# Attention projections on TensorE: tiles of 64 rows and 128 stationary tokens become tiles of 64 rows and 64 stationary tokens, with a semaphore increment ahead of each unit

## The reference

```python
def phi(x):                                   # x: (4, 8, 576, 64), w_phi: (64, 128)
    proj = np.einsum('bhsd,df->bhsf', x, w_phi)
    proj = proj - np.max(np.abs(proj), axis=-1, keepdims=True)
    return np.concatenate([np.exp(proj), np.exp(-proj)], axis=-1)
q_p, k_p = phi(q), phi(k)
kv = np.einsum('bhsf,bhsd->bhfd', k_p, v); z = np.sum(k_p, axis=2)
out = einsum(q_p, kv) / (einsum(q_p, z) + 1e-6)
```

## Time and profile before

| | |
|---|---|
| median of 3 runs | 886.59 us |
| the 3 runs | 884.9, 886.59, 886.87 us |
| span of the profiled execution | 885.2 us |
| PE busy in it | 98% |
| VectorE, ScalarE, GpSimd busy | 63%, 49%, 34% |
| attention, groups in steady state | one every 10.90 us, until about 174 us |

### The profile page before, as it was taken

How to read it: one execution, slowest core, us unless ns; L and a number is a source line. 1 busy time by engine, 2 the same in 40 slices (tenths; PEclk the granted TensorE clock), 3 DMA queues, 4 the chain that set the end, 5 groups by cost and what they waited for, 6 DMA issues and landing times.

```text
span 885.2 us, 19077 instructions
## 1 busy us (share of the span) xinstructions
PE 869.3 (98%) x6818; PEld 790.1 (89%) x6819; DVE 559.7 (63%) x837; ACT 433.4 (49%) x793; POOL 298.6 (34%) x264
## 2 busy tenths in 40 slices
PE   7999999989999999999999999999999999999997
PEld 6888888878888888888888899999999999999997
DVE  4777777798704699930370145642568998778882
ACT  5566666553333443434433656655666743333430
POOL 5687776624435545554352210000000011111111
PEclk9999999989999999999999999999999999999999
DMA  5555555416712587551210037645467644444421
GB/s 140 170 157 156 157 155 154 129 29 213 263 49 97 187 259 247 183 156 58 71 47 32 17 94 204 187 117 142 122 196 203 190 145 142 130 133 119 143 73 48
DMA packets 126677, 122.01 MB, mean 138 GB/s; under 512 B 35040, under 2 KB 101728, under 8 KB 126624
## 3 DMA queue, kind: packets, MB, share of 16 engines
q1 hardware_dynamic: 119088, 103.15, 40.0%
q0 software_dynamic: 3504, 11.28, 4.0%
q10 hardware_dynamic: 4032, 6.86, 2.1%
HBM read 86.39 MB, written 34.88 MB: 137 GB/s over the span
## 4 chain that ended last, share of the span: by engine, by line
PE 94%; DVE 2%; SPq 1%; POOL 1%; DMA 1%; issue 0%; ACT 0%; POOLq 0%; DVEq 0%
PE bank L730 24%; PE bank L728 24%; PE bank L729 24%; PE bank L803 4%; PE bank L742 4%; PE bank L756 3%; PE bank L961 3%; PE bank L723 2%; PE bank L783 1%; PE bank L931 1%; PE bank L1000 1%; PE bank L776 1%; PE bank L765 1%; PE bank L905 1%; PE bank L759 1%
## 5 line engine op out<-in xcount | busy, mean ns | idle before, releaser
L711 POOL DMA_INDIRECT out<-temps,ids x18 | 25.1, 1396 | 324.1 <-DVE temps L1650 321.7
L683 POOL TENSOR_TENSOR h_lo<-h_raw,h_hi 128x512 fp32r<-128x512 f32 x49 | 77.8, 1608 | 126.3 <-ACT h_hi L1218 126.3
L728 PE MATMUL bank<-ops,place 128*128 128x384 f32 (+1 forms) x357 | 119.1, 334 | 0.0
L730 PE MATMUL bank<-ops,place 128*128 128x384 f32 (+1 forms) x357 | 118.3, 331 | 0.0
L729 PE MATMUL bank<-ops,place 128*128 128x384 f32 (+1 forms) x357 | 118.3, 331 | 0.0
L1712 DVE TENSOR_TENSOR temps<-temps,bank 128x384 f32<-128x384 f32 x72 | 39.6, 553 | 73.9 <-PE bank L730 73.8
L728 PE MATMUL bank<-place,ops 128*128 128x256 f32 x294 | 83.2, 283 | 0.0
L729 PE MATMUL bank<-place,ops 128*128 128x256 f32 x294 | 83.2, 283 | 0.0
L730 PE MATMUL bank<-place,ops 128*128 128x256 f32 x294 | 83.2, 283 | 0.0
L1621 DVE CAST w_hi<-ahead 128x1024 fp32r<-128x1024 f32 x48 | 52.3, 1089 | 45.1 <-PE bank L730 45.0
L728 PE MATMUL bank<-w_hi,h_hi 128*128 x200 | 80.4, 402 | 0.2 <-issue 0.2
(11 more groups left out here) (251 smaller groups left out, 2168.3 us busy)
## 6 DMA issues: line engine op xcount, KB each, us to landing
ahead<-in_moe_w SPq DMA_DIRECT2D x56, 512.0 KB, 4.5
h_rows<-temps SPq DMA_DIRECT2D x96, 192.0 KB, 2.5
w_raw<-h_rows SPq DMA_DIRECT2D x17, 512.0 KB, 4.1
y_sorted<-y ACTq DMA_DIRECT2D x25, 256.5 KB, 3.2
raw<-h_rows SPq DMA_DIRECT2D x10, 512.0 KB, 3.7
tail<-h_rows SPq DMA_DIRECT2D x9, 512.0 KB, 3.7
qk<-in_k SPq DMA_DIRECT2D x16, 256.0 KB, 3.3
vs<-in_v SPq DMA_DIRECT2D x16, 256.0 KB, 2.9
```

The lines of the kernel that those rows point to most:

```text
L683: nc.gpsimd.tensor_tensor(h_lo[:, fs, :], h_raw[:, fs, :], h_hi[:, fs, :].bitcast(F32), ALU.subtract).then_inc(h_lo_done, 1)
L728: mm(o, left_hi, right_hi, start=first, stop=False, skip_group_check=shared)
L730: return mm(o, left_lo, right_hi, start=False, stop=last, skip_group_check=shared)
```

## The change

`project` splits each matmul in two by the stationary tokens: tokens 0 to 63 and 64 to 127 are now separate matmuls that write to partitions 0 to 63 and 64 to 127 of the same bank. A unit is 12 matmuls of tile 64*64 (24 records), four of which have four different places of the array. In front of each unit stands an increment of a new semaphore, `proj_begun`, for which nobody waits. The waits that stood before the first matmul now stand before this increment. Between the increment and the first matmul is a wait on the constant 32 for `wphi_loaded`, now in every unit. The results, their places and everything on the other engines stay as they are.

```diff
+        proj_begun = sem("proj_begun")
...
                 pe.wait_ge(xT_moved, UNITS * n + u + 1)
-                if isinstance(n, int) and n == 0 and u == 0:
-                    pe.wait_ge(wphi_loaded, 32)
                 if not (isinstance(n, int) and UNITS * n + u < 2):
                     pe.wait_ge(shift_done, UNITS * n + u - 1)
+                nc.tensor.sem_inc(proj_begun, 1)
+                pe.wait_ge(wphi_loaded, 32)
                 for j in range(PER_UNIT):
-                    for half in range(2):
-                        rows = slice(64 * half, 64 * (half + 1))
-                        last = mm(bank[:, unit_banks(npar, u)[half], j * F:(j + 1) * F],
-                                  xT[rows, PER_UNIT * u + j, :], w_phi2[rows, :], start=True, stop=True)
+                    for m in range(2):
+                        tokens = slice(64 * m, 64 * (m + 1))
+                        for half in range(2):
+                            rows = slice(64 * half, 64 * (half + 1))
+                            last = mm(bank[tokens, unit_banks(npar, u)[half], j * F:(j + 1) * F],
+                                      xT[rows, PER_UNIT * u + j, tokens], w_phi2[rows, :], start=True, stop=True)
                 last.then_inc(proj_done, 1)
```

## The result

| | before | after |
|---|---|---|
| median (18 runs each) | 887.15 us | 885.10 us |
| lowest and highest | 884.9, 888.74 | 882.78, 887.7 |
| profiled execution: time, span | span 885.2 | 885.49, span 883.5 |

The ratio is 0.9972, with a 95% interval of 0.9965 to 0.998: faster by 2.5 us, between 1.8 and 3.1. The medians differ by 2.05 us and the two spans by 1.7 us. The forecast range holds and so does the sign of the forecast, but its size doesn't: it was 0.7 us, and 0.28% is above the 0.2% that can be told from no change. The result is that of the case "more than forecast".

A forecast was written before the change was run, and what follows sets the result against it. PE, busy throughout each 10.90 us attention group, was taken as the bound. 16 groups x 0.05 us = 0.8, less 0.01 us a group, gives 0.7 us: 886.59 - 0.7 = 885.9 us, range 884.2 to 891.5.

The forecast's parts named there:

- more than forecast: Rival, 12%: unit 1's four tiles start close together and it gains 0.08 us too; 2.0 us in all, 884.5 us.
- Four tiles abreast: Projection unit: 24 records run in six steps; a queued unit takes 0.61 us instead of 0.66 from start to last record.
- the 0.05 us of weight loading: Start of a unit: loading 64 instead of 128 tokens shortens the load ahead of the first step, 0.05 us per unit.
- unit 2 counted: Unit 2 stands alone before TensorE's transposes, so its 0.05 us moves everything after it.
- unit 0 waited away: Unit 0's 0.05 us counts nothing: unit 1 is already held 0.05 to 0.08 us by VectorE.
- the increment hidden and not holding the queue: Before each unit: 0.05 us hidden by 0.6 and 0.4 us of run-ahead; rival of a held queue, 896 us, 7%.
- The later end of the last record: End of a unit: four tiles' last record ends later, 0.01 us a group taken off the gain.
- Two abreast: Rival, 10%: hardware doesn't look past blocked records to the fourth tile; twelve steps a unit, 27 us slower, 913 us.
- a group under 10.8 us: Stated sign of being wrong: a group of attention under 10.8 or over 11 us, where 10.85 was expected.
- It gains nothing, or at best 0.08: Unit 1, straight out of a wait: 0.70 us as now with tiles 0.04 us apart; 0.08 us gained if spacing is short.
- the path gains no link: Unit 1: the increment takes over the wait for VectorE that already has its own semaphore instruction; no time added.
- since it only adds work: Increments, 48 in all: a gain from one more semaphore instruction on TensorE's sequencer is excluded.

The follow-up runs named there:

- experiment 3: Kernel after with the token halves in the outer loop, six matmuls of one half before six of the other: group 11.289 us, 893.57 us in one run.
- waits_const: Kernel before (old 64*128 tiles, no increment) with only the constant `wphi_loaded` wait added in every unit: group 10.859 us against 10.900.
- tiles_32: Kernel after with eight tiles of 64*32 instead of four of 64*64: ratio 1.0042 to the kernel before, groups alternating between 10.87 and 11.14 us.
- inc_again: Second measurement of inc_only, the same kernel unchanged: ratio 0.9988 (0.9979 to 0.9997) to the kernel before, group 10.858 or 10.859 us.
- inc_only: Kernel after with the old 64*128 tiles, so increment and moved waits alone: ratio 1.0007 (0.9998 to 1.0015) to the kernel before, group 10.859 us.

## Why the prediction was right in sign and small in size

**What held.** Four tiles abreast (0.618 us measured, 0.61 forecast); the 0.05 us of weight loading as the gain; unit 2 counted, unit 0 waited away in front of VectorE's subtraction; the increment hidden and not holding the queue. The later end of the last record was 0.017 us where I had 0.01. From unit 2 I had 0.04 us a group and it is 0.033. Two abreast, 27 us slower, did not come. By the rule of strict program order (the Trainium skill, "TensorE: Matmul & The Clock Gate", section "Part 3: Packing small matmuls") it would have: these tiles don't follow it, though experiment 3 shows that there is a limit to how far the hardware looks ahead.

**A sign of being wrong that came.** The prediction names a group under 10.8 us as the sign that it is wrong, and the group is 10.773. The time lies in the range, but two steps that lead to it do not hold.

**First step that failed: "It gains nothing, or at best 0.08", unit 1.** I took the 0.04 us between two tiles out of a wait for a spacing that repeats between four. Only the first gap is that long; the next two are 0.007 us, as in a queued unit. Unit 1 gained 0.050 us like the others, 0.75 to 0.8 us over the kernel.

**Second step that failed: "the path gains no link".** That was right for a link more and blind to a shorter one. I costed the increment, which the diff shows, and called a gain excluded, "since it only adds work"; I did not ask what else the instruction with VectorE's wait would hold. It now holds a wait that is met already ahead of VectorE's, and lets go 0.045 us sooner by the records, 0.041 by the group, 0.66 us over the kernel. waits_const has it without the increment.

**The sum.** Forecast 0.05 x 16 less the tail, 0.7 us. Measured 0.127 x 15 + 0.2 = 2.1 us from the groups, 2.05 by medians, and 2.5 (1.8 to 3.1) by the ratio. The rival "more than forecast" had the right size, 2.0 us, but by half of the reason: it gave unit 1 0.08 us, and knew nothing of the wait.

**What stays open.** Why a wait that stands second in its instruction is let go 0.045 us sooner than one that stands alone; and some 0.4 us between the 2.1 of the groups and the 2.5 of the ratio, which its interval also allows to be nothing.

## What to carry to other kernels

Cut small matmuls into tiles only down to where the moving columns still set the step, put matmuls for different places of the array directly behind each other, and keep one form of tile from unit to unit. Where TensorE waits for another engine on the critical path, look at which waits share an instruction, and keep increments behind that wait away. Judge changes of 0.1 us a turn by the period of the loop in the trace, over several turns in a row (tiles_32 alternates between two): its median repeats to 0.002 us where the totals spread over 4.

## What the hardware showed that I had not expected

- Out of a wait, four tiles begin at 0, 0.036, 0.043 and 0.050 us: only the first gap is long.
- A semaphore increment on TensorE's sequencer costs 0.150 us where nothing hides it, while a semaphore instruction that doesn't wait has a record of 51 ns.
- A wait for VectorE that stands second in a semaphore instruction, behind one that is met, starts the weights 0.071 us after VectorE's end, against 0.116 where it stands there alone; constants or registers make no difference.
- A change of the form of tile costs 0.20 us from last record to next weights.
- Look-ahead past blocked records has a limit: tiles of the other token half started after 6 of the 12 records ahead of them.
- Whether a 1.2 GHz stretch follows the mostly idle stretch behind attention differs between executions of one kernel: granted clock 1.00 in inc_again, 0.76 in inc_only over the same window.
- With 48 records a unit instead of 24, every second group is 0.27 us longer, and a loop branch that started 0.2 us into the unit starts 0.6 us into it.
